# Thresholded attention with two dense layers: query halves scaled by 2^-20, the threshold accumulated by the first pass over the scores

## The reference

```python
scores = scale * np.matmul(q, k.transpose(0, 1, 3, 2))       # scale = 1/8
thresh = np.max(scores, axis=-1, keepdims=True) - tau        # tau = 0.02
scores = np.where(scores >= thresh, scores, -1000000000.0)
scores = scores - np.max(scores, axis=-1, keepdims=True)
attn = np.exp(scores)
attn = attn / (np.sum(attn, axis=-1, keepdims=True) + 1e-09)
x = np.matmul(attn, v)                                       # heads side by side: 2304 x 512
# layer 1: h = x @ w_in;  x = (h - tanh(h)) @ w_out
# layer 2: h = x @ w_in;  x = (h * sigmoid(h)) @ w_out
```

## Time and profile before

| | |
|---|---|
| median of 3 runs | 1152.49 us (1151.92 to 1152.94) |
| profiled execution | 1151.28 us, span 1149.5 us |
| TensorE busy, whole span | 1111.5 us (97%) |
| VectorE | 584.7 us (51%) |
| ScalarE | 397.2 us (35%) |
| GpSimd | 264.2 us (23%) |
| granted TensorE clock, mean | 1.00 of full speed |

### The profile page before, as it was taken

One profiled execution on the slowest core, in us unless ns is written; L12 is line 12 of the kernel. 1 busy time (PEld: TensorE's weight loads), 2 busy tenths in 40 slices (PEclk: granted clock), 3 DMA queues, 4 the chain that ended last, 5 costly groups with the idle time before them and its releaser, 6 DMA issues.

```text
span 1149.5 us, 15339 instructions
## 1 busy us (share of the span) xinstructions
PE 1111.5 (97%) x5744; PEld 939.5 (82%) x5744; DVE 584.7 (51%) x1164; ACT 397.2 (35%) x814; POOL 264.2 (23%) x240
## 2 busy tenths in 40 slices
PE   4899999999999999999999999999999999999998
PEld 3778878788788888888888889978888888888898
DVE  7889899898884764334334334462222221231232
ACT  5687776776874322112112111243211111111111
POOL 3565565655644430000000000064200000000000
PEclk9999999999999999999999999999999999999999
DMA  3422324224213320000000000043010000000010
GB/s 98 99 75 73 97 61 99 74 64 95 72 54 112 108 74 1 1 1 0 0 0 0 0 0 1 1 130 109 19 37 1 1 36 0 0 36 0 1 38 19
DMA packets 15193, 48.46 MB, mean 42 GB/s; under 512 B 2080, under 2 KB 2592, under 8 KB 15136
## 3 DMA queue, kind: packets, MB, share of 16 engines
q1 hardware_dynamic: 15136, 47.72, 15.1%
HBM read 42.99 MB, written 4.72 MB: 42 GB/s over the span
## 4 chain that ended last, share of the span: by engine, by line
PE 72%; DVE 1%; ACT 1%; DMA 0%; SPq 0%; issue 0%; POOL 0%; DVEq 0%; ACTq 0%
PE hid L792 34%; PE acc L808 34%; PE pv L710 2%; PE tps L771 1%; PE scores L745 1%; DMA q_raw<-q_in 0%; DVE x_lo L632 0%; ACT w_parts L464 0%; SPq L285 0%; ACT probs L435 0%; POOL q_parts L373 0%; ACT k_hi L446 0%; ACT pT L421 0%; DVE probs L566 0%; DVE pR L596 0%
## 5 line engine op out<-in xcount | busy, mean ns | idle before, releaser
L792 PE MATMUL hid<-x_hi,w_parts 128*128 128x512 f32 (+1 forms) x1280 | 385.4, 369 | 2.1 <-DVE x_lo L632 2.1
L808 PE MATMUL acc<-g_hi,w_parts 128*128 128x512 f32 (+1 forms) x1280 | 384.6, 368 | 0.0
L792 PEld LDWEIGHTS hid<-x_hi,w_parts 128*128 128x128 f32 x1280 | 234.3, 189 | 42.6 <-DVE x_lo L632 2.2
L808 PEld LDWEIGHTS acc<-g_hi,w_parts 128*128 128x128 f32 x1280 | 234.4, 189 | 39.7
L792 PE MATMUL hid<-x_lo,w_parts 128*128 128x512 f32 (+1 forms) x640 | 235.9, 369 | 0.0
L808 PE MATMUL acc<-g_lo,w_parts 128*128 128x512 f32 (+1 forms) x640 | 235.7, 368 | 0.0
L646 DVE CAST g_hi<-h_act 128x512 fp32r<-128x512 f32 (+1 forms) x160 | 71.5, 447 | 267.1 <-ACT h_act L488 264.4
L386 POOL TENSOR_TENSOR w_parts<-w_raw,w_parts 128x1024 fp32r<-128x1024 f32 x30 | 73.6, 2455 | 401.9 <-ACT w_parts L464 401.9
L641 DVE TENSOR_TENSOR h_act<-hid,h_act 128x512 f32<-128x512 f32 (+1 forms) x80 | 51.1, 638 | 205.2 <-ACT h_act L485 205.2
L710 PE MATMUL pv<-pT,v_all 128*128 128x288 f32 x512 | 145.6, 409 | 5.0 <-issue 4.9
L485 ACT ACTIVATE h_act<-hid 128x512 f32<-128x512 f32 (+1 forms) x80 | 44.4, 555 | 294.3 <-PE hid L792 294.3
(11 more groups left out here) (46 smaller groups left out, 795.3 us busy)
## 6 DMA issues: line engine op xcount, KB each, us to landing
w_raw<-w_in SPq DMA_DIRECT2D x32, 512.0 KB, 3.6
k_raw<-k_in SPq DMA_DIRECT2D x30, 288.0 KB, 4.1
q_raw<-q_in SPq DMA_DIRECT2D x30, 288.0 KB, 5.5
v_all<-v_in SPq DMA_DIRECT2D x16, 448.0 KB, 3.5
out<-xT SPq DMA_DIRECT2D x4, 1024.0 KB, 4.2
k_raw<-k_in SPq DMA_DIRECT2D x4, 144.0 KB, 2.9
q_raw<-q_in SPq DMA_DIRECT2D x4, 144.0 KB, 2.8
out<-xT SPq DMA_DIRECT2D x1, 512.0 KB, 2.9
```

The source lines that it names most:

```text
L792: last = pe.matmul(hid[f % HBANKS][:, 0:w], a, b[:, kc, 0:w], start=(kc == 0 and i == 0), stop=(kc == KC - 1 and i == 2))
L808: last = pe.matmul(acc[n][:, 0:w], a, b[f % GRING][:, 0:w], start=(f == 0 and i == 0), stop=(f == FT - 1 and i == 2))
```

## The change

- The queries are scaled by 2^-20 when they are split. ScalarE's copy of the high part gets the scale. In front of each low part GpSimd scales the raw queries in place (a new operation on 128 x 576), and the low part waits for that. This scaling stands ahead of the normalization of its step. In the very first pair VectorE scales and subtracts in one `scalar_tensor_tensor`.
- The scores so come out of TensorE already multiplied by 2^-20. The first pass subtracts `margin` (tau times 2^-20 over the scale, at most that of 110) and accumulates the maximum of the result, which is the threshold `thr` itself.
- The lift follows the first pass (and L575, in the steps that have it) and uses `thr`. The operation on `stats` is gone. Behind the lift stands a `tensor_scalar` on 128 x 1 that computes `exp_bias`, and the exponential waits for it too.
- The copy L596 and the reciprocal L604 keep their code, but now stand behind the lift and the bias.
- The set-up of tau has fewer small operations.

```diff
-UNMASKED = 3.0e38
+UNMASKED = 2.0 ** 40
+DEEPEST = 110.0
@@ gpsimd, steps()
                 for k in ks:
+                    what, h = split_in(k - 1, first)
+                    g, u = PAIRS * B + k // TILES, k // TILES % 2
+                    if what == "queries":
+                        pool.wait_ge(q_hi_done, 2 * g + h + 1)
+                        rows = q_raw[:, h]
+                        pool.tensor_scalar(rows, rows, FINE, 1.0, ALU.mult, ALU.mult).then_inc(q_fine, 1)
                     q = k - L_NORM
                     if here(q):
...
-                    what, h = split_in(k - 1, first)
-                    g, u = PAIRS * B + k // TILES, k // TILES % 2
                     if what == "queries":
-                        pool.wait_ge(q_hi_done, 2 * g + h + 1)
+                        pool.wait_ge(q_fine, 2 * (g - 1) + h + 1)
@@ scalar, steps()
                         act.wait_ge(lift_done, n + 1)
-                        act.activation(tile, tile, ACT.Exp, bias=stats[:, c, 0:1], scale=-SCALE / FINE,
+                        act.wait_ge(bias_done, n + 1)
+                        act.activation(tile, tile, ACT.Exp, bias=exp_bias[:, c:c + 1], scale=-SCALE / FINE,
                                        accum_out=rowsum[:, c:c + 1]).then_inc(exp_done, 1)
...
-                        act.activation(q_parts[u][:, h, 0:SEQ], q_raw[:, h], ACT.Copy).then_inc(q_hi_done, 1)
+                        act.activation(q_parts[u][:, h, 0:SEQ], q_raw[:, h], ACT.Copy, scale=FINE).then_inc(q_hi_done, 1)
@@ vector, tau
-            dve.tensor_scalar(fine[:], tau_ok[:], FINE, None, ALU.mult)
-            dve.memset(stat_scale[:, 0:1], -SCALE / FINE)
-            dve.memset(stat_scale[:, 1:2], 1.0 / FINE)
-            dve.memset(stat_bias[:, 0:1], 0.0)
-            dve.tensor_scalar(tau_low[:], tau_ok[:], UNMASKED, -UNMASKED, ALU.mult, ALU.add)
-            dve.tensor_scalar(margin[:], tau[:], -1.0 / SCALE, tau_ok[:], ALU.mult, ALU.mult).then_inc(tau_steps, 1)
+            dve.tensor_scalar(tau_low[:], tau_ok[:], -UNMASKED, UNMASKED, ALU.mult, ALU.add)
+            dve.tensor_scalar(tau_high[:], tau[:], DEEPEST, FINE / SCALE, ALU.min, ALU.mult).then_inc(tau_steps, 1)
             dve.wait_ge(tau_steps, 2)
-            dve.tensor_tensor(stat_bias[:, 1:2], margin[:], tau_low[:], ALU.add).then_inc(tau_steps, 1)
+            dve.tensor_tensor(margin[:], tau_high[:], tau_low[:], ALU.max).then_inc(tau_steps, 1)
@@ vector, steps()
-                        dve.tensor_scalar(tile, scores[q % SBUFS][:, :, 0:HALF], fine[:], None, ALU.mult, ALU.max,
-                                          accum_out=finemax[:, c:c + 1]).then_inc(max_done, 1)
+                        dve.tensor_scalar(tile, scores[q % SBUFS][:, :, 0:HALF], margin[:], None, ALU.subtract,
+                                          ALU.max, accum_out=thr[:, c:c + 1]).then_inc(thr_done, 1)
...
                     q = k - L_S
                     if here(q):
                         n, c = STEPS * B + q, q % RING
-                        dve.wait_ge(max_done, n + 1)
-                        dve.scalar_tensor_tensor(out=stats[:, c], in0=stat_scale[:], scalar=finemax[:, c:c + 1],
-                                                 in1=stat_bias[:], op0=ALU.mult,
-                                                 op1=ALU.add).then_inc(stats_done, 1)
+                        dve.wait_ge(thr_done, n + 1)
+                        tile = probs[:, slot_of(q), :].rearrange("p (a s) -> p a s", a=2)
+                        dve.scalar_tensor_tensor(out=tile, in0=scores[q % SBUFS][:, :, 0:HALF],
+                                                 scalar=thr[:, c:c + 1], in1=tile, op0=ALU.is_lt,
+                                                 op1=ALU.subtract).then_inc(lift_done, 1)
+                        dve.tensor_scalar(exp_bias[:, c:c + 1], thr[:, c:c + 1], -SCALE / FINE, None,
+                                          ALU.mult).then_inc(bias_done, 1)
...
-                    q = k - L_S
-                    if here(q):
-                        n, c = STEPS * B + q, q % RING
-                        dve.wait_ge(stats_done, n + 1)
-                        tile = probs[:, slot_of(q), :].rearrange("p (a s) -> p a s", a=2)
-                        dve.scalar_tensor_tensor(out=tile, in0=scores[q % SBUFS][:, :, 0:HALF],
-                                                 scalar=stats[:, c, 1:2], in1=tile, op0=ALU.is_lt,
-                                                 op1=ALU.subtract).then_inc(lift_done, 1)
@@ vector, splits of the first pair
-                dve.tensor_tensor(rows, q_raw[DH:P, h], rows.bitcast(F32), ALU.subtract).then_inc(qk_split, 1)
+                dve.scalar_tensor_tensor(out=rows, in0=q_raw[DH:P, h], scalar=FINE, in1=rows.bitcast(F32),
+                                         op0=ALU.mult, op1=ALU.subtract).then_inc(qk_split, 1)
```

More of the change, by code:

```diff
@@ L176, in build @@
         tau_ok = sb("tau_ok", [P, 1])
-        fine = sb("fine", [P, 1])
-        stat_scale = sb("stat_scale", [P, 2])
-        stat_bias = sb("stat_bias", [P, 2])
         tau_low = sb("tau_low", [P, 1])
+        tau_high = sb("tau_high", [P, 1])
         margin = sb("margin", [P, 1])
-        finemax = sb("finemax", [P, RING])
-        stats = sb("stats", [P, RING, 2])
+        thr = sb("thr", [P, RING])
+        exp_bias = sb("exp_bias", [P, RING])
         rowsum = sb("rowsum", [P, RING])
@@ L244, in build @@
         scores_done = sem("scores_done")
-        max_done = sem("max_done")
-        stats_done = sem("stats_done")
+        q_fine = sem("q_fine")
+        thr_done = sem("thr_done")
+        bias_done = sem("bias_done")
         exp_done = sem("exp_done")
@@ L452, in _ @@
                 act.activation(k_hi[0][:, h], k_raw[:, h], ACT.Copy).then_inc(k_hi_done, 1)
-                act.activation(q_parts[0][:, h, 0:SEQ], q_raw[:, h], ACT.Copy).then_inc(q_hi_done, 1)
+                act.activation(q_parts[0][:, h, 0:SEQ], q_raw[:, h], ACT.Copy, scale=FINE).then_inc(q_hi_done, 1)
             steps(0, range(STEPS), True)
```

## The result

The changed kernel is slower: 1163.38 us, median of 4 runs (1161.18 to 1163.90), against 1152.72 (4 runs, 1151.92 to 1153.54). The ratio is 1.0091, 95% interval 1.0079 to 1.0103, so 10.7 us between the medians. The forecast was 1171.1 us, 18.6 us slower. The profiled execution took 1163.38 us with a span of 1161.6.

The account below looks back on a forecast made before the run. The prediction took a loop over k_hi, VectorE's reciprocal, GpSimd's second query split and the next load as the bound. 14 loops x 1.20 = 16.8, first pair 1.1, end 0.7, start 0: 18.6 us slower, 1171.1; range 1158 to 1175.

Parts of the forecast that it names:

- the weaker case: Attention loop costs less than forecast: 1165.6 us if VectorE and GpSimd miss each other, 1160.9 if the copy is harmless too; chance 0.20.
- The loop: Attention stage, per head pair: k_hi to second query split 11.73, split 1.41, load to next k_hi 7.34; 20.48 us.
- Copy behind the lift, TensorE gated by it, scores of j7 late: Attention pair: copy to pR 0.69 us later delays TensorE's one-tile transpose and j7's scores; j7's pass starts 0.10 later.
- The collision: VectorE's L575 for j7 falls inside GpSimd's second query scaling and is held to its end; 0.39 us a loop.
- The weaker rival's first form: L575 and the second scaling miss each other, copy still gates j7: 0.81 us a loop, 1165.6 us; rival's chance 0.20.
- Reciprocal behind the lift: Attention loop: lift and bias before the reciprocal, less the removed stats operation, make it 0.71 us later.
- Scalings hidden: GpSimd's two query scalings per pair fill time it waited for rinv; uncovered they would cost 2 x 0.73 us.
- First pair: GpSimd runs its splits back to back there, so the two scalings may be uncovered: 1.1 us taken.
- End: Last pair: the late copy to pR still gates TensorE, which carries the delay into the dense stage; 0.7 us.
- Start: First two query splits on VectorE become scalar_tensor_tensor and keep 0.76 us each; 0 added.
- Faster, VectorE's total is the limit: Attention stage: load wait is only slack, so each removed stats operation pays; 18 us gained, 1134.5 us; chance 0.10.
- No change: Gain of the plain steps just outweighs the late reciprocal, with copy and collision harmless: 1152 us; chance 0.06.

Follow-up runs that it names:

- a_recip: The changed kernel with the reciprocal alone moved back ahead of the lift; 1157.79 us, 1.0043 to the kernel before.
- b_kearly: The kernel before with a pair's key load waiting only for the key splits, not the second query split; 1138.94 us, 0.9887.
- b_recip: The kernel before with only the reciprocal moved behind the lift; 1163.71 us, 1.0107.
- a_noscale: The changed kernel without GpSimd's two query scalings per pair and the wait for them, a timing probe only; 1159.48 us, 1.0060.
- a_copy: The changed kernel with the copy to pR alone ahead of the lift, the reciprocal still behind it; 1158.35 us, 1.0057.
- a_both: The changed kernel with both the copy to pR and the reciprocal ahead of the lift; 1152.47 us, 0.9999.

## Why the prediction was right in its direction and too high in its size

The time lies in my range of 1158 to 1175 only because the range took in the weaker case. The forecast itself, 1168 to 1174 with a chance of 0.64, missed; what came is the weaker case, to which I gave 0.20.

- *The loop* stands. Its three parts were found again in the changed kernel, the wait for the load is unchanged, and the load's early start took 12.6 us from the kernel before.
- *Copy behind the lift, TensorE gated by it, scores of j7 late*: right. The copy came 0.52 later than before, not 0.69, and j7's pass 0.06 earlier, not 0.10 later. The term that was mis-sized is the small operation: I let one pass in 0.11 us, from the stats row. The bias passes in 0.06 (171.79 to 171.85) and the reciprocal in 0.08 (170.15 to 170.23), so each place in the queue came some hundredths earlier than I had it, and j7's pass 0.16.
- *The collision* is the step that failed, and the largest error: 0.39 of the 1.20 us per loop. In 12 of the 14 loops it did not take place. L577 started at 175.29, 0.15 earlier than I had it (with 4.72 subtracted), and took 0.16; the scaling started at 175.46, 0.19 later than I had it, since it starts 0.83 behind a normalization (170.52 to 171.35) and not the 0.73 that I took, and two of these stand in the way. L577 slipped in at the normalization's end (174.63 + 0.75 = 175.38). My two starts were 0.17 us apart the other way round, so whether they met was luck. In the 2 other loops GpSimd ran 0.3 us later, L577 met the normalization, as I had written against the weaker rival, and the loop took 0.17 more:

```profile
196.35 0.74 POOL L365 TENSOR_SCALAR probs<-probs,rinv 128x576 f32<-128x576 f32 x1 [0.20 <-POOL q_parts L378]
```

```profile
196.71 0.40 DVE L577 TENSOR_SCALAR rowsum_e<-rowsum 128x3 f32<-128x3 f32 x1
```

  The weaker rival's first form (collision missed, copy still gating j7) is what happened; it gave 0.81 a loop, and the loop measured 0.61. The size of a hold was near right: 0.28 us in a_recip for a start 0.25 into the scaling, where I took 0.39 for 0.17. The Trainium skill's rule (SBUF — State Buffer, "SBUF: two separate sides") agrees with this and with the 1.45 us of b_kearly's stats operation; what it can't give is whether two instructions meet.
- *Reciprocal behind the lift*: right. It now comes 1.66 us behind the start of its step's pass (174.55 to 176.21), before 0.99 (169.89 to 170.88), so 0.67 for the predicted 0.71. With the earlier pass: 0.67 - 0.06 = 0.61, times 14 is 8.5 for 16.8. a_recip and b_recip show the cause by moving the reciprocal alone.
- *Scalings hidden*: nearly right for the loops, as the changed kernel has them (0.1 each by a_noscale). But they are covered only by the delay of VectorE that the new order makes: in a_copy and a_both, where VectorE is sooner, GpSimd's queue with the scalings in it sets the split.
- *First pair*: right, 1.2 for 1.1, and by the mechanism that I gave, the scalings in the open.
- *End*: 0.5 for 0.7. *Bias*: never held, see below. *Exponential's wait*: 0, as taken; ScalarE stood idle before its exponentials for 0.3 us in all from 36 to 320 us (0.4 before).
- *Start*: 0, as taken, from VectorE's timeline at the start (0.76 before):

```profile
7.77 0.76 DVE L618 SCALAR_TENSOR_TENSOR q_parts<-q_raw,q_parts 64x576 fp32r<-64x576 f32 x1
```

  The Trainium skill (Vector Engine (DVE) Microarchitecture Reference, "Points that are easy to get wrong") has this operation at half rate with two fp32 sources in SBUF. The trace disagrees: 0.76 us, as the tensor_tensor of the same shape in the kernel before. The measurement decides.
- *Faster, VectorE's total is the limit*: ruled out by a_both, which has the lighter VectorE and gains nothing. It becomes true only with the loop opened (13.65 us). *No change*: ruled out too; the time stays only in a_both, with both moves undone, and that is another condition than the one I gave it (a harmless copy and no collision).

The sum by measured terms is 1.2 + 8.5 + 0.5, with 0.2 for loads that took longer: 10.4 us, for 10.5 measured. The 8.1 us that the forecast had too much lie almost wholly in the loops (8.5 for 16.8): about 5.1 in the collision, the rest in the small operations.

## What to carry to other kernels

Where a buffer is loaded again only after its last reader, follow that loop over all engines before pricing an edit: what delays an instruction inside it is paid in every turn, and what is saved outside it turns into waiting. On an engine that works in order, an operation whose result the loop waits for belongs ahead of the long pass that can come later; here two such places, a reciprocal of 0.17 us and a copy of 0.68, cost 10.7 us, and mending only one gave half. Where a forecast hangs on whether two operations 0.2 us apart meet, give both outcomes a real chance. A saving on one engine becomes visible only when loop and order allow it: the same arithmetic was worth nothing, and 13.65 us with the key load released early.

## What the runs showed of the hardware

- The bias operation, a tensor_scalar on a 128x1 tile, was never held beside GpSimd. Groups of 36 to 320 us in the changed kernel:

```profile
L588 DVE TENSOR_SCALAR exp_bias<-thr 128x1 f32<-128x1 f32 x120 | 17.2, 143 | 0.0
```

  All 144 of the kernel took 136 to 147 ns, 56 of them wholly inside a GpSimd operation. A 128x3 tensor_scalar took 0.54 us and a 128x2 scalar_tensor_tensor 1.45 us in such a place. Nor was the 128x3 reciprocal: in a_copy 12 of them lay wholly inside GpSimd's scaling and took 0.16 to 0.17 us, as elsewhere. So the size alone doesn't decide. What does was not tried.
- GpSimd's tensor_scalar in place (q_raw onto itself) took 673 ns on average, that of the normalization with its scalar from a tile 746 ns, at the same 128x576.
- After the same gap on TensorE, between the two layers, one execution was granted 0.57 and 0.80 and another 1.00. What decides between them stays open.
